# The second product of a ReLU-squared layer by tile pairs: half of its depth plainly, half as seven quarter products

## The chip, the cores and the metric

One core of a Trainium2 chip. The metric is the device time of one execution in microseconds (us). In the text TensorE is PE (its weight loads PEld), VectorE is DVE, ScalarE is ACT, GpSimd is POOL, and SP is the engine whose queue starts most transfers.

## What is computed

Windowed attention with sinks, then a layer with a gated softmax and a normalization, then a last layer. The change touches the last layer:

```python
def _moe2_ref(x, w_in, w_out):        # x 1536 x 512, w_in 512 x 2048, w_out 2048 x 512
    h = x @ w_in
    r = np.maximum(h, 0.0)
    g = r * r
    return (g @ w_out).astype(np.float32)   # the second product
```

Everything is fp32, to be kept nearly exactly. A product of two fp32 matrices is made of three matmuls in the format fp32r: each operand is split into a rounded part (hi) and the rest (lo), and hi x hi, hi x lo and lo x hi are summed in PSUM.

## The kernel before

The kernel runs on hand-written queues: each engine has its own list of instructions, in the order of the program text of its block, and semaphores tie them together. There is no scheduler; whatever stands behind a waiting instruction of the same engine waits too.

The attention and the middle layer take the first 200 us. Then comes the first product of the last layer, transposed: `g` has the shape [128, NJ = 8, 2, 1536], where chunk (j, r) is the 128 rows 128 x (8r + j) of `g` transposed. The first two j are made of plain quarters (`quarter`), the six others (`multiply`, j = 2 to 7) as seven products each with 384 columns: the scheme multiplies a 2 x 2 block matrix with seven products instead of eight, at the price of sums of blocks. Each of these seven products is 12 matmuls. DVE adds its results (`sum_2`, `sum_3`, `lower_right`, `lower_left`, `upper_right`), ACT copies two of them (`copy_p1`, `corner`), and DVE applies max and square (`gate_row`, L1559). POOL sums and splits the weights of that product (L791 to L805) and has nothing to do after it.

The second product, `project2` (L2014 to L2034), takes 12 tiles of 128 tokens. For a tile t, the 16 chunks of `g` are the stationary operand, and `wy`, the split w_out, the moving one, with 512 columns: 16 x 3 = 48 matmuls add up one PSUM bank. ACT rounds a whole tile of g (`round_g`, L1141) into one of two buffers `g_hi`, DVE subtracts to get `g_lo` (`split_g`, L1573), two tiles ahead. The eight pairs of chunks of w_out are loaded, rounded by ACT (`round_wy`, L1132) and split by DVE (`split_wy`, L1563) around the change from the first product to the second. The first two tiles are done in turns of four chunks, so that TensorE can begin before all of `wy` is there. Finished banks are copied by ACT (even tiles) or DVE (odd ones) into `y`, and SP stores them. The last tile's bank is copied by DVE in two halves (L1581, L1582), the second of which ACT's own queue stores (L1212).

TensorE's operand order is plain there:

```python
for k in range(3):
    gs, w = ((g_hi, 0), (g_hi, 1), (g_lo, 0))[k]
    done = mm(y_ps[t % 8], gs[t % 2][:, n, :], wy[n // 2][:, n % 2, w, :], ...)
```

## Time and profile before

| | us |
|---|---|
| median of 3 runs | 476.38 (475.81 to 476.69) |
| the profiled execution | 474.66 |
| its span, first to last instruction | 472.9 |
| TensorE busy | 462.9 |
| VectorE busy | 303.9 |
| ScalarE busy | 213.7 |
| GpSimd busy | 126.0 |
| granted TensorE clock, mean | 0.999 |

The profile is one execution, so times inside it are compared with its own 474.66. A matmul's recorded duration contains its way through the array; successive matmuls overlap, and what a matmul costs in a stream is the distance between starts. Loads of weights (PEld) overlap matmuls. The same holds, to a smaller degree, for the other engines: an instruction starts some 0.08 us before the record of the one before it ends. In a line of the timeline "x2" means that two like instructions are shown as one, from the first start to the last end. Idle time of an engine that is not on the chain costs nothing.

### The profile page before, as it was taken

Reading aid. Unit: us, or ns where it says so; the run is one execution under the profiler, and the core shown is the slowest. Engines: PE = TensorE matmul, PEld = TensorE weight load, DVE = VectorE, ACT = ScalarE, POOL = GpSimd, SP = SyncE. Lnnn points to the kernel's source line nnn. Section 1 sums busy time; section 2 is a strip of 40 time slices with the busy share of each in tenths; the row PEclk is TensorE's granted clock in tenths of the full one; section 3 lists DMA queues with packets and bytes.
Section 4 is the critical chain, followed back from the end, with each engine's and each line's share of the span. In section 5 each row is a group of like instructions: output and inputs, shape, how many; then the busy total and the mean of one; then the engine's idle time right before and its main releaser. Section 6 shows DMA issues by size and latency. Waiting matters only on the chain.

```text
span 472.9 us, 7375 instructions
## 1 busy us (share of the span) xinstructions
PE 462.9 (98%) x2754; PEld 395.4 (84%) x2754; DVE 303.9 (64%) x491; ACT 213.7 (45%) x538; POOL 126.0 (27%) x175
## 2 busy tenths in 40 slices
PE   8889999999999999999999999999999999999997
PEld 6667787887778887788999999999988888888885
DVE  3899888998898889874863766557974121212120
ACT  4687777656866576444554122222533212122210
POOL 2366333231311330512444576551000000000000
PEclk9999999999999999999999999999999999999999
DMA  7921124543564855464301111011511000000010
GB/s 225 326 85 48 52 71 138 169 126 78 162 169 130 189 134 156 110 152 117 91 1 46 44 46 46 0 44 49 191 73 45 23 22 24 22 24 22 22 46 22
DMA packets 60443, 41.87 MB, mean 89 GB/s; under 512 B 28344, under 2 KB 48056, under 8 KB 60408
## 3 DMA queue, kind: packets, MB, share of 16 engines
q1 hardware_dynamic: 59640, 40.74, 30.7%
q10 hardware_dynamic: 768, 0.66, 0.5%
q8 instruction: 22, 0.36, 0.3%
q14 instruction: 13, 0.11, 0.1%
HBM read 30.38 MB, written 11.01 MB: 88 GB/s over the span
## 4 chain that ended last, share of the span: by engine, by line
PE 90%; DVE 3%; POOL 3%; ACT 2%; issue 1%; DVEq 0%; POOLq 0%
PE wo_ps L1816 13%; PE h_ps L1776 12%; PE wt_ps L2031 9%; PE score_ps L2031 9%; PE score_ps L1978 7%; PE h_ps L2010 5%; PE score_ps L2010 5%; PE wo_ps L2031 5%; PE h_ps L2031 5%; PE wo_ps L2010 4%; PE wt_ps L2010 4%; PE wo_ps L1738 3%; PE score_ps L1704 3%; PE wt_ps L1704 1%; POOL pT_own L697 1%; PE wt_ps L1715 1%
## 5 line engine op out<-in xcount | busy, mean ns | idle before, releaser
L1573 DVE TENSOR_TENSOR g_lo<-g,g_hi 128x2048 fp32r<-128x2048 f32 (+2 forms) x14 | 27.7, 1986 | 76.4 <-ACT g_hi L1141 75.2
L1141 ACT ACTIVATE g_hi<-g 128x2048 fp32r<-128x2048 f32 (+2 forms) x14 | 23.3, 1671 | 84.9 <-PE score_ps L2031 25.2
L2031 PE MATMUL wt_ps<-wy,g_hi 128*128 128x512 f32 x128 | 39.7, 391 | 0.0
L2031 PE MATMUL score_ps<-wy,g_hi 128*128 128x512 f32 x128 | 39.7, 391 | 0.0
L882 ACT ACTIVATE prob<-sm,nbias 128x132 f32<-128x132 f32 (+1 forms) x96 | 37.7, 394 | 3.7 <-DVE nbias L1231 3.0
L1816 PE MATMUL wo_ps<-wo_hi,lnT_hi 128*128 128x512 f32 x88 | 36.1, 411 | 0.0
L1776 PE MATMUL h_ps<-w_hi,xT_hi 128*128 128x512 f32 x88 | 35.3, 401 | 0.8 <-DVE xT_lo L1340 0.5
L1816 PE MATMUL wo_ps<-wo_hi,lnT_lo 128*128 128x512 f32 x88 | 35.0, 398 | 0.0
L1776 PE MATMUL h_ps<-w_hi,xT_lo 128*128 128x512 f32 x88 | 34.5, 392 | 0.0
L1816 PE MATMUL wo_ps<-wo_lo,lnT_hi 128*128 128x512 f32 x88 | 34.4, 391 | 0.0
L1776 PE MATMUL h_ps<-w_lo,xT_hi 128*128 128x512 f32 x88 | 34.3, 390 | 0.0
L805 POOL TENSOR_TENSOR w_lo<-w_raw,w_hi 128x512 fp32r<-128x512 f32 x16 | 22.1, 1386 | 41.7 <-ACT w_hi L1110 41.7
L2031 PEld LDWEIGHTS wt_ps<-wy,g_hi 128*128 128x128 f32 x128 | 24.0, 188 | 5.2
L2031 PEld LDWEIGHTS score_ps<-wy,g_hi 128*128 128x128 f32 x128 | 24.0, 188 | 5.1
L2031 PE MATMUL wt_ps<-wy,g_lo 128*128 128x512 f32 x64 | 25.1, 392 | 0.0
L2031 PE MATMUL score_ps<-wy,g_lo 128*128 128x512 f32 x64 | 25.0, 390 | 0.0
L687 POOL CAST p_sink<-prob 128x64 fp32r<-128x64 f32 x10 | 4.8, 484 | 75.2 <-DVE prob L1307 75.2
L1559 DVE SCALAR_TENSOR_TENSOR g<-g 128x1536 f32<-128x1536 f32 x12 | 22.9, 1914 | 0.3
L1776 PEld LDWEIGHTS h_ps<-w_hi,xT_hi 128*128 128x128 f32 x88 | 16.5, 188 | 6.8 <-issue 3.5
L1978 PE MATMUL score_ps<-xc_hi,w_hi 128*128 128x384 f32 x64 | 21.5, 337 | 0.0
L1978 PE MATMUL score_ps<-xc_lo,w_hi 128*128 128x384 f32 x64 | 21.5, 336 | 0.0
L1978 PE MATMUL score_ps<-xc_hi,w_lo 128*128 128x384 f32 x64 | 21.5, 336 | 0.0
(231 smaller groups left out, 1263.0 us busy)
## 6 DMA issues: line engine op xcount, KB each, us to landing
u_dram<-uT SPq DMA_DIRECT2D x18, 256.0 KB, 3.3
lnT_raw<-u_dram SPq DMA_DIRECT2D x36, 128.0 KB, 2.8
w_raw<-w_in SPq DMA_DIRECT2D x16, 256.0 KB, 3.3
V<-v SPq DMA_DIRECT2D x12, 256.0 KB, 3.3
wy_in<-w_out SPq DMA_DIRECT2D x6, 512.0 KB, 4.0
x_dram<-x SPq DMA_DIRECT2D x44, 64.0 KB, 2.2
out<-y SPq DMA_DIRECT2D x11, 256.0 KB, 2.0
k_raw<-kT SPq DMA_DIRECT2D x20, 132.0 KB, 2.8
```

What stands on the lines that cost most here:

```text
L805: nc.gpsimd.tensor_tensor(w2_slots(w2_lo[j % 2], part), w2_part(j, part), w2_slots(w2_hi[j % 2], part).bitcast(F32), ALU.subtract).then_in ...
L882: nc.scalar.activation(prob[:, h, seen(n)], sm[:, h, seen(n)], ACT.Exp, bias=nbias[:, h:h + 1], scale=-1.0 if alone(n) else SCALE, accum_o ...
L1141: nc.scalar.activation(g_hi[t % 2][:, chunks, :], g_tile(t, chunks), ACT.Copy).then_inc(g_rounded, 1)
L1559: nc.vector.scalar_tensor_tensor(h, h, 0.0, h, ALU.max, ALU.mult).then_inc(g_ready, 1)
L1573: nc.vector.tensor_tensor(g_lo[t % 2][:, chunks, :], g_tile(t, chunks), g_hi[t % 2][:, chunks, :].bitcast(F32), ALU.subtract).then_inc(g_s ...
L1704: done = mm(score_banks(n, p)[:, j, cols], qs[rows], ks[rows], start=(n < 2 or i == 0), stop=(n < 2 or i == len(products) - 1))
L1738: last = mm(o_ps[rows, cols], V[:, slot, h * D:(h + 1) * D], pT[:, g, j * P:(j + 1) * P], start=(g == 0 and part == 0 and i < 2 and not si ...
L1776: done = mm(h_ps[:, cols], xs[:, c, :], ws[:, c, cols], start=(c == 0 and k == 0), stop=(c == MC - 1 and k == 2))
L1816: done = mm(x2_bank(t)[:, :], ls[:, k, :], ws[:, k, :], start=(k == 0 and i == 0), stop=(k == C1 - 1 and i == 2))
L1978: done = mm(quarter_ps[n % 2], ws[j % 2][:, 2 * r + half, cc, :], x(s, xs[half])[:, cc, :], start=(c == 0 and k == 0), stop=(c == MC - 1 a ...
L2010: last = mm(prod_pairs[j % 2][bank][:, s, 0:TH], ws[j % 2][:, wk, c, :], xs[s][xk][:, c, :], start=(opens and c == 0 and k == 0), stop=(c ...
L2031: done = mm(y_ps[t % 8], gs[t % 2][:, n, :], wy[n // 2][:, n % 2, w, :], start=(n == 0 and k == 0), stop=(n == C2 - 1 and k == 2))
```

## The change

The 12 tiles become 6 pairs (p, p + 6). The depth of the product, the eight j, is cut in two.

- The *plain* part of a pair uses j = 0 to 3: four items of 12 matmuls with 512 columns (two tiles x two halves of the chunks), into the pair's two banks `pair_ps[p % 3]`.
- The *seven* part uses j = 4 to 7. Its matrix is cut into quarters: the two tiles of the pair by the two r, and w_out by r and by halves of 256 columns. Seven items of 12 matmuls with 256 columns (4 chunks x 3). In order: FIFTH, FIRST, THIRD, SIXTH, SECOND, SEVENTH, FOURTH. FIFTH has a bank of its own; FIRST, SIXTH and SEVENTH share one (`chain_ps`), which ACT or DVE must have read before the next may open it; the rest adds onto the plain part's banks.
- The order of the parts (`PLAN`) is plain 0, 1, 2, seven 0, plain 3, seven 1, plain 4, seven 2, seven 3, plain 5, seven 4, seven 5: 24 + 42 = 66 items.
- An item's high part is rounded by ACT into a ring of seven buffers of 512 elements, its low part is written by DVE over g itself; both are made seven items ahead.
- POOL makes the four sums of blocks of g of each pair, S1 to S4, of 512 elements each, after the pair's plain part, over the chunks that the plain part has used. DVE waits for two of them before it splits the pair's FIFTH item, and for all four before FIRST.
- Of w_out, j = 0 to 3 are loaded, rounded and split as before. The rest is loaded as four quarters, DVE makes four differences T1 to T4, ACT rounds seven matrices of 1024 elements and DVE splits them, written between the items 0 to 7.
- Of a seven part ACT copies three results (`keep`), DVE adds the others (`flush`) into `y`; SP stores a tile of the pair when DVE has added the last.

```diff
+PLAN = (("plain", 0), ("plain", 1), ("plain", 2), ("seven", 0), ("plain", 3), ("seven", 1),
+        ("plain", 4), ("seven", 2), ("seven", 3), ("plain", 5), ("seven", 4), ("seven", 5))
+PAIR_PRODUCTS = ((S1, T1), (A11, B11), (S4, B22), (S2, T2), (A12, B21), (S3, T3), (A22, T4))
...
+            def sum_g(p, k):
+
+                done = len(WST_SUMS) * p
+                if k == S1:
+                    pool.wait_ge(item_done, item("plain", p, PARTS - 1) + 1)
+                    pool.wait_ge(g_ready, gates_before(NJ))
+                elif k == S2:
+                    pool.wait_ge(s_summed, done + 1)
+                elif k == S4:
+                    pool.wait_ge(s_summed, done + 2)
...
+                nc.gpsimd.tensor_tensor(g_sum(g, p, k), a, b, op).then_inc(s_summed, 1)
...
                 copy_p1(j)
                 if j == NJ - 1:
-                    round_g(0, 0)
+                    for n in range(6):
+                        round_item(n)
                 corner(j)
...
+            for n in range(len(ITEMS)):
+                keep(n)
+                if n + RING < len(ITEMS):
+                    round_item(n + RING)
+                if n == 0:
+                    round_wst(B11)
...
+            def prepare(n):
+
+                kind, p, i = ITEMS[n]
+                if kind == "seven" and i == FIFTH:
+                    dve.wait_ge(s_summed, len(WST_SUMS) * p + 2)
+                elif kind == "seven" and i == FIRST:
+                    dve.wait_ge(s_summed, len(WST_SUMS) * (p + 1))
+                split_item(n)
...
+                if i == SIXTH:
+                    dve.wait_ge(kept, kept_before(p) + 1)
+                    nc.vector.tensor_tensor(upper[:, HALF:DM], chain_ps, lower[:, HALF:DM], ALU.add).then_inc(chain_summed, 1)
...
+            for n in range(len(ITEMS)):
+                flush(n)
+                if n + RING < len(ITEMS):
+                    prepare(n + RING)
+                if n == 1:
+                    sum_wst(T1)
+                    sum_wst(T2)
+                elif n == 2:
+                    split_wst(T1)
+                    sum_wst(T3)
+                elif n == 3:
+                    sum_wst(T4)
+                    split_wst(B11)
+                elif n == 4:
+                    split_wst(B22)
+                    split_wst(T2)
+                elif n == 5:
+                    split_wst(B21)
+                elif n == 6:
+                    split_wst(T3)
+                elif n == 7:
+                    split_wst(T4)
...
+                elif i == SIXTH:
+                    pe.wait_ge(kept, kept_before(p) + 2)
+                elif i == SEVENTH:
+                    pe.wait_ge(chain_summed, 2 * p + 1)
...
+                for c in range(NJ - PLAIN):
+                    for k in range(3):
+                        gs, w = ((item_high(n), 0), (item_high(n), 1), (item_raw(g_low, n), 0))[k]
+                        done = mm(bank, gs[:, c, :], wst[wk][:, w, c, :], start=((i in (FIFTH, FIRST) or bank is last_ps) and c == 0 and k == 0),
+                                  stop=(c == NJ - PLAIN - 1 and k == 2), skip_group_check=True)
```

## Rows read from the trace of the kernel before

**Rows 1.** The page's first part: busy us, share of the span, instructions.

```profile
PE 462.9 (98%) x2754; PEld 395.4 (84%) x2754; DVE 303.9 (64%) x491; ACT 213.7 (45%) x538; POOL 126.0 (27%) x175
```

**Rows 2.** The chain that ended last: start us, us, what (TensorE's two products).

```profile
250.29 2.09 PE score_ps L2010 x12
...
338.01 21.88 PE score_ps L2031 x96
```

**Rows 3.** Busy time by engine from 349 us to the last matmul.

```profile
349.00:469.90 120.90, 120.88 (x528) 98.76 (x527) 28.63 (x18) 23.17 (x18) 0.00 (x0) 1.00 0.07 24
```

**Rows 4.** Timeline, TensorE, matmuls of 260 columns: start us, us, engine, line.

```profile
109.89 0.39 PE L1704 MATMUL score_ps<-KH,QH 64*128 64x260 f32 x2
110.12 0.28 PE L1704 MATMUL score_ps<-KL,QH 64*128 64x260 f32 x2
...
110.47 0.28 PE L1704 MATMUL wt_ps<-KL,QH 64*128 64x260 f32 x2
```

**Rows 5.** Weight loads: two groups by shape (busy us, mean ns | idle), one timeline line.

```profile
L2031 PEld LDWEIGHTS wt_ps<-wy,g_hi 128*128 128x128 f32 x128 | 24.0, 188 | 5.2
...
L1759 PEld LDWEIGHTS wo_ps<-p_sinkT,v_sink 96*128 96x128 f32 x40 | 5.7, 190 | 1.6 <-issue 0.7 <-ACT p_sinkT L900 0.4
...
125.32 0.52 PEld L1759 LDWEIGHTS wo_ps<-p_sinkT,v_sink 96*128 96x128 f32 x4 [0.39 <-issue]
```

**Rows 6.** Timeline, VectorE, an instruction of 512 elements and the next one.

```profile
9.35 0.69 DVE L1307 TENSOR_TENSOR prob<-prob,rz 128x512 f32<-128x512 f32 x1
9.96 0.69 DVE L1472 TENSOR_SCALAR w_hi<-w_stage 128x1024 fp32r<-128x1024 f32 x1
```

**Rows 7.** Groups by shape: line, engine, shapes, count | busy us, mean ns | idle before.

```profile
L1563 DVE TENSOR_TENSOR wy<-wy_ahead,wy 128x1024 fp32r<-128x1024 f32 x2 | 2.4, 1218 | 0.0
...
L1110 ACT ACTIVATE w_hi<-w_sum 128x512 fp32r<-128x512 f32 x6 | 3.7, 622 | 0.0
...
L1126 ACT COPY g<-h_ps 128x768 f32<-128x768 f32 x3 | 2.4, 804 | 7.1 <-PE h_ps L2010 7.1
```

**Rows 8.** Timeline of VectorE and ScalarE at the change of products.

```profile
337.97 2.02 DVE L1573 TENSOR_TENSOR g_lo<-g,g_hi 128x1792 fp32r<-128x1792 f32 x1
338.10 2.01 ACT L1132 ACTIVATE wy<-wy_ahead 128x1024 fp32r<-128x1024 f32 x2 [1.73 <-PE h_ps L2010]
...
339.91 2.35 DVE L1563 TENSOR_TENSOR wy<-wy_ahead,wy 128x1024 fp32r<-128x1024 f32 x2
...
342.18 0.95 DVE L1545 TENSOR_TENSOR g<-h_ps,g 128x768 f32<-128x768 f32 x1
343.05 3.42 DVE L1559 SCALAR_TENSOR_TENSOR g<-g 128x1536 f32<-128x1536 f32 x2
```

**Rows 9.** One line's instructions, L805: ns min/median/max, first and last start us.

```profile
L805 POOL TENSOR_TENSOR w_lo<-w_raw,w_hi x16: 1284/1298/2029, 196.1 to 319.0; 128x512 fp32r<-128x512 f32 x16
```

**Rows 10.** Timeline, GpSimd and VectorE together, both operands of each in SBUF.

```profile
196.13 1.29 POOL L805 TENSOR_TENSOR w_lo<-w_raw,w_hi 128x512 fp32r<-128x512 f32 x1 [2.19 <-ACT w_hi L1110]
...
196.71 1.53 DVE L1522 TENSOR_TENSOR xc_lo<-x2T,xc_hi 128x768 fp32r<-128x768 f32 x1
...
197.38 2.01 POOL L805 TENSOR_TENSOR w_lo<-w_raw,w_hi 128x512 fp32r<-128x512 f32 x1
...
196.71 3.50 DVE L1522 TENSOR_TENSOR xc_lo<-x2T,xc_hi 128x768 fp32r<-128x768 f32 x2
```

**Rows 11.** Timeline, VectorE reading PSUM beside GpSimd.

```profile
265.76 0.94 DVE L1545 TENSOR_TENSOR g<-score_ps,g 128x768 f32<-128x768 f32 x1
266.40 0.74 POOL L799 TENSOR_TENSOR w_last<-w_raw,w_sum 128x256 f32<-128x256 f32 x1
```

**Rows 12.** Timeline of the end: the last copies and ScalarE's store.

```profile
469.92 0.42 DVE L1581 COPY y<-wt_ps 128x256 f32<-128x256 f32 x1 [17.10 <-PE wt_ps L2031]
470.26 0.41 DVE L1582 COPY y<-wt_ps 128x256 f32<-128x256 f32 x1
...
470.71 0.36 ACTq L1212 DMA_DIRECT2D out<-y  x1
```

More of the change, by code:

```diff
@@ L68 @@
 P_FIRST, P_SECOND, P_CORNER, P_THIRD, P_LOWER, P_LEFT, P_RIGHT = range(NP)
-EARLY_TILES = 2
 AHEAD = (2, 3)
-WY_LOADS = AHEAD + (0, 1, 4, 5, 6, 7)
+PLAIN = 4
+WY_LOADS = AHEAD + (0, 1)
+HALF = DM // 2
+NPAIR = NT // 2
+RING = 7
+PLAN = (("plain", 0), ("plain", 1), ("plain", 2), ("seven", 0), ("plain", 3), ("seven", 1),
+        ("plain", 4), ("seven", 2), ("seven", 3), ("plain", 5), ("seven", 4), ("seven", 5))
+PAIR_PRODUCTS = ((S1, T1), (A11, B11), (S4, B22), (S2, T2), (A12, B21), (S3, T3), (A22, T4))
+FIFTH, FIRST, THIRD, SIXTH, SECOND, SEVENTH, FOURTH = range(NP)
+PARTS = PLAIN
+WST_ROUNDS = (B11, B22, T1, T2, B21, T3, T4)
+WST_SPLITS = (T1, B11, B22, T2, B21, T3, T4)
+WST_SUMS = (T1, T2, T3, T4)
 LN_EPS, SM_EPS = 1e-6, 1e-9
@@ L198, in gates_before, with parts_of, kept_before, item @@
     return len(BLOCKS) + 2 * (j - CLASSIC)
+def parts_of(kind):
+    return PARTS if kind == "plain" else NP
+ITEMS = tuple((kind, p, i) for kind, p in PLAN for i in range(parts_of(kind)))
+def kept_before(p):
+    return 3 * p
+def item(kind, p, i):
+    return ITEMS.index((kind, p, i))
 def seen(n):
@@ L841, in _ @@
                 split_w2(j)
+            for p in range(NPAIR):
+                for k in (S1, S2, S3, S4):
+                    sum_g(p, k)
         @block.scalar
@@ new lines, in round_wst, with keep @@
+            def round_wst(k):
+                if k in WST_SUMS:
+                    act.wait_ge(wst_summed, WST_SUMS.index(k) + 1)
+                else:
+                    act.wait_ge(wst_loaded, 16 * 4)
+                nc.scalar.activation(wst[k][:, 0, :, :], wst_raw(k), ACT.Copy).then_inc(wst_rounded, 1)
+            def keep(n):
+                kind, p, i = ITEMS[n]
+                upper, lower = y[2 * (p % 2)], y[2 * (p % 2) + 1]
+                if kind == "plain" or i not in (FIFTH, FIRST, SEVENTH):
+                    return
+                act.wait_ge(item_done, n + 1)
+                if i == FIFTH:
+                    if p >= 2:
+                        act.wait_ge(y_stored[p % 2], 32 * (p // 2))
+                    nc.scalar.copy(lower[:, HALF:DM], fifth_ps).then_inc(kept, 1)
+                elif i == FIRST:
+                    nc.scalar.copy(upper[:, 0:HALF], chain_ps).then_inc(kept, 1)
+                else:
+                    nc.scalar.copy(lower[:, 0:HALF], chain_ps).then_inc(kept, 1)
@@ L1636, in _ @@
                 if last:
[L1637 removed]
+                    split_item(0)
+                    split_item(1)
                 elif j - CLASSIC + 1 < len(BLOCKS):
@@ L1640, in _ @@
                 sum_3(j)
+                if last:
+                    split_item(2)
                 lower_right(j)
@@ new lines, in plain_part @@
+            def plain_part(p, i):
+                n = item("plain", p, i)
+                half, part = i % 2, i // 2
+                pe.wait_ge(item_split, n + 1)
+                if p == 0 and i == 0:
+                    pe.wait_ge(added, 5 * (NJ - 1 - CLASSIC))
+                elif p == 2 and i == 0:
+                    pe.wait_ge(added, 5 * (NJ - CLASSIC))
+                elif p >= 3 and part == 0:
+                    pe.wait_ge(y_summed, 2 * (p - 3) + half + 1)
+                for c in range(4):
+                    j, r = 2 * part + c // 2, c % 2
+                    if p == 0:
+                        pe.wait_ge(wy_split, j + 1)
+                    for k in range(3):
+                        gs, w = ((item_high(n), 0), (item_high(n), 1), (item_raw(g_low, n), 0))[k]
+                        done = mm(pair_ps[p % 3][half], gs[:, c // 2, r, :], wy[j][:, r, w, :],
+                                  start=(part == 0 and c == 0 and k == 0), stop=(part == 1 and c == 3 and k == 2),
+                                  skip_group_check=True)
+                done.then_inc(item_done, 1)
@@ L2047, in _ @@
                     multiply(j, n)
-            for first, last in ((0, 4), (4, 8), (8, C2)):
-                for t in range(EARLY_TILES):
-                    project2(t, first, last)
-            for t in range(EARLY_TILES, NT):
-                project2(t, 0, C2)
+            for kind, p in PLAN:
+                for i in range(parts_of(kind)):
+                    if kind == "plain":
+                        plain_part(p, i)
+                    else:
+                        seven_part(p, i)
 def kernel(q, k, v, n_sink, window, moe_w_in, moe_w_out, moe_g_ln, moe2_w_in, moe2_w_out):
```

245 lines of the change are left out of this document (151 added, 94 removed).

## The prediction

> **What bounds the kernel now.** I read the page's first part, then the chain that ended last, then the second product's stretch, then the engines beside it. TensorE is busy 98% of 472.9 us, GpSimd 27% [rows 1]. The chain is TensorE alone from 250.29 on, and from 338.01 on it is L2031, the second product, in six pieces of 22 us each [rows 2] up to the last copies at 469.92 [rows 12]. From 349 on TensorE is busy 120.88 of 120.90 us at a granted clock of 1.00 (that is 2.4 GHz), while VectorE works 28.6 us, ScalarE 23.2, GpSimd 0 [rows 3]. So a shorter matmul stream shortens the kernel one for one, as long as the three other engines feed it. Their idle time looks ample as an average; it has to be read block by block.
>
> **TensorE's stream.** Before: 576 matmuls of 512 columns in 131.9 us, 0.229 each. After: six pairs with 48 plain matmuls each (288 of 512 columns), and 84 of 256 columns each (504), where plain work would have been 96 of 256. The trace has no 128-row matmul of 256 columns. In the first product, 504 matmuls of 384 columns go from 250.29 to 338.01: 0.174 each, waits every twelve included [rows 2]. A line through 512 and 384 gives 0.119 at 256. The nearest row agrees: 260 columns in 64 rows, two side by side, go on every 0.117 us (110.12 to 110.47 in three steps) [rows 4]. I take 0.119, bounds 0.117 and 0.174 (384 columns). New stream 288 x 0.229 + 504 x 0.119 = 66.0 + 60.0 = 125.9, so **-6.0 us**. Break-even is 65.9/504 = 0.131.
>
> **Weight loads.** Each narrow matmul comes with its own load of 128x128 weights, as wide a load as a 512-column matmul has. A load is recorded at 0.19, of 128 rows as of 96; but loads overlap: four of 96 rows end within 0.52, so (0.52 - 0.19)/3 = 0.11 apart [rows 5]. 0.119 is just above that; what a narrower margin would do is rival 3.
>
> **What DVE has to do before the first seven-product block.** Prices: splitting 512 elements 0.69 alone, the next instruction starts 0.61 later (9.35 to 9.96) [rows 6]; 1024 elements 1.22, two in 2.35, so 1.13 apart [rows 7, 8]; an addition from PSUM of 768 elements 0.95 [rows 7], so about 0.42 for 256 and 0.36 to the next start. The handover: before, split of g 337.97 to 339.99, two wy splits, addition, two gates to 346.47 [rows 8]. After, the long split is one of 0.61; the wy splits wait for ScalarE's first rounding (half of 2.01, so 339.1) and end at 341.4; addition 342.3; three item splits 344.1; gates 347.4. TensorE doesn't notice: the first items were split during the last block of the first product. ScalarE's six roundings put in ahead of the corner copy cost 6 x 0.62 minus overlap, and end near 330.0; the copy (0.80 [rows 7]) ends 330.9, before the fifth product's start at 331.8 (three products of 2.09 before 338.01). Cover 0.9; it costs that much more if gone. On SP's queue four loads of halves of w_out (512 KB each) take the place of the last four of eight, and twelve stores stay twelve; ScalarE asks for the halves after its first item, DVE after 348.6, some ten us after the last of them may start at 338.0. Cover several us; no cost.
>
> From 347.4 DVE runs in its written order. Before TensorE may open the sixth product of pair 0 (SEVENTH, which waits for DVE's addition of SIXTH out of the shared bank) DVE has: 15 item splits (7 to 21) x 0.61 = 9.1; 4 weight sums and 7 weight splits x 1.13 = 12.4; the addition 0.36. Sum 21.9, so 369.3. TensorE wants it at 338.0 + 144 x 0.229 + 60 x 0.119 = 378.1. **Slack 8.8 us** if GpSimd costs DVE nothing.
>
> **GpSimd's sums.** 24 additions of 512 elements, four per pair: nearest row L805, 512 elements of the same stride pattern, 1.29 median, 2.03 worst [rows 9]. The worst one is the point. At 196.13 GpSimd starts (1.29, ends 197.42); DVE starts a two-input split of 768 at 196.71 and takes 1.53 where 0.95 is usual, ending 198.24: 0.82 after GpSimd. GpSimd's next starts at 197.38, takes 2.01, ends 199.39: 1.15 after DVE. DVE's second ends at 200.21 (196.71 + 3.50), again 0.82 after [rows 10]. They take turns, whole instruction by whole instruction. An addition that reads PSUM doesn't take part: 0.94 beside a GpSimd instruction of its usual 0.74 [rows 11]. So one turn of GpSimd costs a full DVE queue 1.15 + 0.82 - 0.87 = **1.10 us** (0.87: start to start of 768 elements, 342.18 to 343.05 [rows 8]). The Trainium skill (GPSIMD Engine Reference, section Key points) says the two share SBUF interfaces and contend when the Vector instruction has two SBUF inputs; the trace agrees and gives the price, which the page doesn't.
>
> *Block seven 0.* Pairs 0, 1, 2 have their sums released when plain 0, 1, 2 end (349, 360, 371): all 12 fall in DVE's full stretch. 12 x 1.10 = 13.2 against 8.8 of slack: **+4.4 us**. At 1.0 a turn +3.2, at 1.30 +6.8, below 0.73 nothing.
>
> *Blocks seven 1 and seven 2* follow a plain part whose sums are released at the same moment. With 0 there: sum 1.4, split 2.0, sum 3.1, split 3.7, sum 4.8, split 5.4, sum 6.5, split 7.05, addition of SIXTH 7.45; TensorE wants it at 5 x 1.43 = 7.15. **+0.3 each** (0 to 1.2). *Seven 3* has no sums beside it. *Seven 4*: DVE's split for pair 5's FIRST waits for all four sums of pair 5 (queued behind that wait on DVE: the later splits and seven 4's own addition of SIXTH, on which TensorE waits). Sums end 6.0, two splits 7.3, addition 7.7: **+0.6** (0.3 to 1.5).
>
> After a stop the first matmul comes on 0.23 instead of 0.12 later (109.89, 110.12 [rows 4]): 0.11 x 4 = **+0.4**. DVE's additions otherwise replace copies of similar length, with 22 us of slack per pair.
>
> *Tail.* Before: two DVE copies in a row (469.92, 470.26 for 0.41), then ScalarE issues the store at 470.71 [rows 12], 0.8 after the last matmul. After: one addition, ready when the last product ends or up to 0.3 later (ScalarE copy, then 0.42 and 0.69 behind SEVENTH, against 1.43). **-0.1** (-0.3 to +0.3).
>
> **Sum.** -6.0 + 4.4 + 0.3 + 0.3 + 0.6 + 0.4 - 0.1 = -0.1 us on the profiled execution: 474.66 (span 472.9, 1.7 around it) to 474.6. That execution is 1.7 below the median of the three runs, 476.38, within the few tenths of a per cent by which runs differ; on the median the forecast is **476.3 us**: no change that can be measured (0.2% is 0.95 us, about what a measurement of this kernel can tell).
>
> **Rivals.**
> 1. *The turns cost little* (GpSimd's sums slip in where DVE waits anyway, or a waiting GpSimd instruction is passed over until DVE stops). For it: GpSimd isn't needed early for pairs 1 and 2. Against: rows 10. With 0.9 a turn, seven 0 stops 2.0 and the later ones vanish: -6.0 + 2.0 + 0.2 - 0.1, 472.5; with none, -6.1: 470.3.
> 2. *The turns cost more: slower.* Place: seven 0. If a turn costs the whole 1.30, stops are 6.8 + 1.2 + 1.2 + 1.5, restarts 0.4: +5.0, 481.4; half way +2.5, 478.8. It decides from a turn of 1.19 on (12 x 0.09 more than forecast). For it: dependent sums wait for each other's semaphores. Against: between two sums DVE has a turn, which covers that.
> 3. *Narrow matmuls are bound by their loads: slower.* If a load of 128 rows went on in proportion to rows, 0.11 x 128/96 = 0.147: 504 x 0.147 = 74.1, +8.2 against before, partly under the stops: +9, 485. Against: a load of 96 rows and one of 128 are recorded alike, 190 and 188 ns [rows 5]. The Trainium skill (TensorE: Matmul & The Clock Gate, section LDWEIGHTS) says that a load's time goes by its columns alone, 107 ns for 128, which no row here shows for 128 rows; by it this rival falls away.
> 4. *The change doesn't do what it says*: that the rewritten stream isn't run as written (say both halves still plain) is excluded by the diff; that the weights' halves come late to pair 0 is inside the forecast, since their eleven instructions stand in the same DVE queue and their stop is the one counted. No chance of its own.
>
> **How the numbers follow.** Forecast case 0.50 (474.8 to 478.0 on the median; of it 0.14 faster, 0.25 same, 0.11 slower); rival 1 0.27, all faster; rival 2 0.18, slower; rival 3 0.05, slower. Faster 0.41, same 0.25, slower 0.34. The range reaches into rival 1 down to 471.2 and into rival 2 up to 479.8, leaving about 0.1 at either end.
>
> **What would show it.** Steps right: 512-column matmuls every 0.229 and 256-column ones every 0.119; DVE nearly unbroken from 347 to 382, its splits stretched from 0.69 to 1.8 wherever GpSimd runs; TensorE idle about 4 us within the first seven-product block, waiting on DVE, a few tenths in the second, third and fifth, none in the fourth. Wrong: GpSimd's sums waiting long and bunched (rival 1), TensorE's narrow matmuls at 0.13 or more without waits (rival 3), a granted clock that drops during the stops.

## The result, and the profile after

The changed kernel takes 478.0 us in the median (476.62 to 480.29, 12 runs), the kernel before 475.94 (474.81 to 477.26, 12 runs). The ratio is 1.0045, with a 95% interval of 1.0028 to 1.0063: slower by 2.1 us, where no change was forecast. The profiled execution of after took 479.0 us (span 477.2), that of before 474.66 (span 472.9).

Of the 4.3 us between those two spans, 2.1 lie ahead of the second product, whose first matmul starts at 337.84 us in the trace of before and at 339.96 in that of after. That is no effect of the change: in the fifteen traces of this study that moment lies anywhere from 337.75 to 339.96, and the lowest is that of e7 below, which differs from after only inside the second product. So from here on I compare L, the time from the first matmul start of the second product to the last. It is 131.65 us before and 134.0 after. With the tail (last matmul start to the end of the span, 3.43 and 3.27) that makes +2.2 us, against +2.1 by the medians.

The page's line of engine times, which answers [rows 1]:

```profile
PE 460.7 (97%) x2970; PEld 403.2 (84%) x2970; DVE 356.5 (75%) x568; ACT 235.6 (49%) x605; POOL 167.6 (35%) x199
```

TensorE has 2.2 us less work, and is the bound for a smaller share. Busy time by engine, as in [rows 3], from 349 us to the last matmul, and then within the first seven-product block (columns: PE, PEld, DVE, ACT, POOL, each with its count; granted clock; DMA share; GB/s):

```profile
349.00:474.20 125.20, 119.78 (x754) 107.61 (x752) 83.82 (x95) 45.44 (x80) 41.78 (x24) 1.00 0.06 24
372.90:387.90 15.00, 11.03 (x85) 10.23 (x84) 14.37 (x17) 5.24 (x10) 7.72 (x4) 1.00 0.05 17
```

TensorE idles 5.4 us in the first of these, 4.0 of them in the block, where VectorE is busy 14.4 of 15.0. (A matmul's record reaches into the gap behind it, so idle time by records is a little under the stops by starts that I give below.) The granted clock is 1.00 (2.4 GHz) all along. The waits from 335 us to the end put the idle time on VectorE (engine, line, waited for: us, times, longest):

```profile
PEld wo_ps L2245 <- DVE g_low L1692: 6.3, 5, 2.4
...
PE wo_ps L2245 <- DVE y L1733: 3.2, 4, 1.7
```

The chain that ended last, which answers [rows 2], is no longer TensorE alone. It runs through VectorE's weight sums and splits and then its item splits (start us, us, what):

```profile
358.14 2.32 DVE wst_in L1715
366.18 4.56 DVE wst L1720 x2
...
379.74 4.78 DVE g_low L1692 x6
388.12 11.20 PE score_ps L2214 x48
...
409.95 11.20 PE wt_ps L2214 x48
```

TensorE at the entry of block seven 0 and at its two large stops (timeline):

```profile
372.92 0.40 PE L2245 MATMUL wo_ps<-wst,ring 128*128 128x256 f32 x2
373.15 0.28 PE L2245 MATMUL wo_ps<-wst,g_low 128*128 128x256 f32 x1
...
379.87 0.50 PE L2245 MATMUL wo_ps<-wst,ring 128*128 128x256 f32 x2 [2.20 <-DVE g_low L1692]
...
385.01 0.47 PE L2245 MATMUL wo_ps<-wst,ring 128*128 128x256 f32 x2 [1.74 <-DVE y L1733]
```

By the starts of all narrow matmuls between two stops they come every 0.120 us (the first two take 0.23 here, 372.92 to 373.15): [rows 4] was a good neighbour. The stops are in the block that the forecast named. Split over the block by the starts of the matmuls they are 0.19, 2.36, 0.16 and 1.90: 4.6 us. They stand ahead of THIRD, SIXTH, SECOND and SEVENTH. The forecast had all of it ahead of SEVENTH; more than half comes two items earlier, where SIXTH waits for its own low part, which stands in the same late VectorE queue.

VectorE and GpSimd in the stretch before (timeline), which answers [rows 6] and [rows 10]:

```profile
351.19 8.19 POOL L896 TENSOR_TENSOR g<-g 128x512 f32<-128x512 f32 x4 [28.09 <-PE score_ps L2214]
...
354.19 1.78 DVE L1692 TENSOR_TENSOR g_low<-g,ring 128x512 fp32r<-128x512 f32 x1
355.90 2.31 DVE L1720 TENSOR_TENSOR wst<-wst_in,wst 128x1024 fp32r<-128x1024 f32 x1
358.14 2.32 DVE L1715 TENSOR_TENSOR wst_in<-wst_in,wst_in 128x1024 f32<-128x1024 f32 x1
360.38 0.68 DVE L1692 TENSOR_TENSOR g_low<-g,ring 128x512 fp32r<-128x512 f32 x1
```

Beside GpSimd, a split of 512 takes 1.71 from start to start (354.19 to 355.90) where alone it takes 0.61, and one of 1024 takes 2.24 (355.90 to 358.14) where alone it takes 1.13. The differences are 1.10 and 1.11: a turn costs the same whatever VectorE's instruction is, and costs what the forecast said. The block's sum holds too. VectorE ended the gates at 349.68, and its addition of SIXTH at 384.86:

```profile
346.26 3.42 DVE L1681 SCALAR_TENSOR_TENSOR g<-g 128x1536 f32<-128x1536 f32 x2
...
384.45 0.41 DVE L1733 TENSOR_TENSOR y<-wo_ps,y 128x256 f32<-128x256 f32 x1
```

That is 35.2 us; the forecast had 21.9 of work and 13.2 of turns, 35.1.

What the forecast didn't have is in the plain parts. Two rows of plain 1, ahead of any narrow block, and two of plain 3, which follows block seven 0; in each pair the second starts six matmuls after the first:

```profile
360.33 0.39 PE L2214 MATMUL wt_ps<-wy,g_low 128*128 128x512 f32 x1
...
361.70 0.39 PE L2214 MATMUL wt_ps<-wy,g_low 128*128 128x512 f32 x1
...
396.12 0.40 PE L2214 MATMUL score_ps<-wy,g_low 128*128 128x512 f32 x1
...
397.52 0.40 PE L2214 MATMUL score_ps<-wy,g_low 128*128 128x512 f32 x1
```

Six matmuls of 512 columns take 1.37 us ahead of the first narrow block and 1.40 behind it. Over all 144 on either side that is 0.229 each (32.96 us by the starts) against 0.2333. The chain says the same with all 48 of a part: 11.20 us, where 96 of before took 22.00 and so 48 took 11.0. All three plain parts that follow a narrow block run so, 144 matmuls; the three ahead of it run at 0.229.

Blocks seven 1, seven 2 and seven 4 stop once each, at the same place, ahead of SEVENTH. VectorE's addition of SIXTH in seven 1, the same in seven 4, and TensorE behind the latter:

```profile
406.29 0.41 DVE L1733 TENSOR_TENSOR y<-wo_ps,y 128x256 f32<-128x256 f32 x1
...
460.49 0.42 DVE L1733 TENSOR_TENSOR y<-wo_ps,y 128x256 f32<-128x256 f32 x1
...
461.05 0.47 PE L2245 MATMUL wo_ps<-wst,ring 128*128 128x256 f32 x2 [0.79 <-DVE y L1733]
```

By the starts of the matmuls the stops are 0.49 (seven 1), 0.49 (seven 2) and 0.95 (seven 4), and none in seven 3 and seven 5. The tail, which answers [rows 12]:

```profile
474.57 0.42 DVE L1746 TENSOR_TENSOR y<-score_ps,y 128x256 f32<-128x256 f32 x1
475.03 0.36 ACTq L1334 DMA_DIRECT2D out<-y  x1
```

### The profile page after: what moved, and what is told of

Its sections match the earlier page's. It is cut to its first block, busy times and chain, and to the rows that moved or that the text cites. A ratio compares the mean times of both kernels' runs of the same rounds, so it can differ in the third digit from the quotient of the medians.

```text
span 477.2 us, 8100 instructions
## 1 busy us (share of the span) xinstructions
PE 460.7 (97%) x2970; PEld 403.2 (84%) x2970; DVE 356.5 (75%) x568; ACT 235.6 (49%) x605; POOL 167.6 (35%) x199
## 4 chain that ended last, share of the span: by engine, by line
PE 68%; DVE 14%; DMA 5%; POOL 4%; issue 4%; SPq 3%; ACT 2%; POOLq 0%; DVEq 0%; ACTq 0%
PE h_ps L1959 10%; PE wo_ps L1999 10%; PE score_ps L2161 7%; PE h_ps L2193 5%; PE score_ps L2193 5%; PE wo_ps L2245 5%; PE wo_ps L2193 4%; PE wt_ps L2193 4%; DVE g_low L1692 4%; PE h_ps L2214 2%; PE wt_ps L2214 2%; PE score_ps L2214 2%; PE wo_ps L1921 2%; DVE wst L1720 2%; DMA V<-v 2%
## 5 line engine op out<-in xcount | busy, mean ns | idle before, releaser
L1692 DVE TENSOR_TENSOR g_low<-g,ring 128x512 fp32r<-128x512 f32 x66 | 57.2, 881 | 31.8 <-ACT ring L1239 29.0
L896 POOL TENSOR_TENSOR g<-g 128x512 f32<-128x512 f32 x24 | 41.8, 1762 | 94.2 <-PE score_ps L2214 46.5
L1239 ACT ACTIVATE ring<-g 128x512 fp32r<-128x512 f32 x66 | 40.5, 629 | 49.3 <-PE h_ps L2214 14.6
L2245 PE MATMUL wo_ps<-wst,ring 128*128 128x256 f32 x192 | 35.7, 285 | 5.4 <-DVE y L1733 3.2
L1959 PE MATMUL h_ps<-w_hi,xT_hi 128*128 128x512 f32 x88 | 35.2, 400 | 1.5 <-DVE xT_lo L1462 1.2
L2245 PEld LDWEIGHTS wo_ps<-wst,ring 128*128 128x128 f32 x192 | 30.1, 191 | 6.6 <-DVE g_low L1692 6.3
L2245 PE MATMUL wo_ps<-wst,g_low 128*128 128x256 f32 x96 | 27.1, 283 | 0.0
L1000 ACT ACTIVATE e<-h_ps,nhmax 128x512 f32<-128x512 f32 x24 | 16.3, 685 | 10.8 <-DVE nhmax L1383 10.7
L2214 PE MATMUL wt_ps<-wy,ring 128*128 128x512 f32 x64 | 20.1, 395 | 0.0
```

The costliest lines, as they stand in the source:

```text
L896: nc.gpsimd.tensor_tensor(g_sum(g, p, k), a, b, op).then_inc(s_summed, 1)
L1239: nc.scalar.activation(item_high(n), item_raw(g, n), ACT.Copy).then_inc(item_rounded, 1)
L1692: nc.vector.tensor_tensor(item_raw(g_low, n), item_raw(g, n), item_high(n).bitcast(F32), ALU.subtract).then_inc(item_split, 1)
L1959: done = mm(h_ps[:, cols], xs[:, c, :], ws[:, c, cols], start=(c == 0 and k == 0), stop=(c == MC - 1 and k == 2))
L2214: done = mm(pair_ps[p % 3][half], gs[:, c // 2, r, :], wy[j][:, r, w, :], start=(part == 0 and c == 0 and k == 0), stop=(part == 1 and c = ...
L2245: done = mm(bank, gs[:, c, :], wst[wk][:, w, c, :], start=((i in (FIFTH, FIRST) or bank is last_ps) and c == 0 and k == 0), stop=(c == NJ ...
```

## The experiments

My theory after the result: GpSimd's sums take 1.10 us each from VectorE's queue; this stops TensorE 6.5 us, and 0.6 us more go to restarts behind the stops (the first matmuls of a product that comes after a stop stand 0.07 to 0.1 further apart). Without the stops the new order of work gains what its matmuls give. Rivals: the seven-product blocks are slow for a reason of their own (weights late, banks, order), or GpSimd's sums are themselves the late operand. Each kernel is the kernel after with the edit shown, unless it says otherwise. Ratios are against the kernel before, run beside it. This is what came out:

| kernel | median us | ratio (95%) | L, us | stops, us |
|---|---|---|---|---|
| after | 478.0 | 1.0045 (1.0028 to 1.0063) | 134.0 | 4.6, 0.49, 0.49, 0.95 |
| e1 sums of 1 element | 470.96 | 0.9893 (0.9874 to 0.9912) | 126.91 | none |
| e2 sums of 256 | 470.92 | 0.9892 (0.9869 to 0.9914) | 126.91 | none |
| e7 sums of 384 | 471.88 | 0.9927 (0.9902 to 0.9952) | 128.64 | 1.67 |
| e8 copies of 512 | 470.98 | 0.9909 (0.9893 to 0.9925) | 126.91 | none |
| e5 sums on VectorE | 471.19 | 0.9905 (0.9879 to 0.9931) | 126.91 | none |
| e3 sums released later | 472.64 | 0.993 (0.9911 to 0.9948) | 128.54 | 0.55, 0.94 |
| e4 later, other plan | 471.31 | 0.992 (0.9888 to 0.9951) | 127.53 | 0.54 |
| e9 short weight splits | 472.99 | 0.9945 (0.9932 to 0.9959) | 129.61 | 0.49, 0.49, 0.49, 0.95 |
| e6 each sum twice | 498.98 | 1.0491 (1.0463 to 1.052) | 154.83 | 20.2 in all |

**e1: GpSimd's sums cut to one element.** The splits of the items that would read a sum read g itself.

```diff
-                nc.gpsimd.tensor_tensor(g_sum(g, p, k), a, b, op).then_inc(s_summed, 1)
+                nc.gpsimd.tensor_tensor(g_sum(g, p, k)[:, 0:1, 0:1], a[:, 0:1, 0:1], b[:, 0:1, 0:1], op).then_inc(s_summed, 1)
```

> Leaves out the pairs' sums of g: each of GpSimd's 24 instructions works on one element per partition instead of 512, and the items that used the sums take a quarter of g in their place (same sizes, same waits). Theory 1 (turns: GpSimd's two-input instructions and VectorE's with both inputs in SBUF take turns, 1.1 us each, which makes VectorE's queue late): all stops of TensorE in the four blocks (4.6, 0.5, 0.5, 0.95 us) and their restarts (0.5) vanish, the 512-element splits are back at 0.69 us: 478.0 - 7.0 = 471.0, ratio to the kernel before 0.990. Rival A (VectorE's own queue, 11 weight instructions and 15 splits, is too long, GpSimd or not): the stops in the first block stay, 477 or more. Rival B (ScalarE's roundings come late): as rival A.

470.96 us, and every stop is gone: L is 126.91. All of the 7.1 us between this and after (134.0 - 126.91) hang on the length of GpSimd's sums; with short sums, weights, banks and the order of the plan stop TensorE nowhere. The plain parts behind narrow blocks stay at 0.2333, so that has nothing to do with the length of GpSimd's sums.

**e2 and e7: 256 and 384 of the 512 elements.** Does the price go by the size of GpSimd's instruction? As in e1, the items that would read a sum read g. The edit of e2 (e7 has 96 in place of P // 2):

```diff
-                nc.gpsimd.tensor_tensor(g_sum(g, p, k), a, b, op).then_inc(s_summed, 1)
+                nc.gpsimd.tensor_tensor(g_sum(g, p, k)[:, :, 0:P // 2], a[:, :, 0:P // 2], b[:, :, 0:P // 2], op).then_inc(s_summed, 1)
```

> As the run with one element, but each of GpSimd's sums covers 256 of the 512 elements (so half of each sum is left out). Theory 1: a turn of 256 elements costs VectorE 0.55 us, 12 x 0.55 = 6.6 us are less than the 8.8 us of slack before the first seven-product block's SEVENTH, so no stop there, and at most 0.1 to 0.3 in the last: 471.0 to 471.4, the same as with one element. A rival in which the loss goes in proportion to GpSimd's work (bandwidth of the memory shared by all instructions, say) gives half of the loss: 474.5.

> As the runs with shortened sums, but 384 of the 512 elements (a quarter of each sum left out). Theory 1: a turn costs VectorE (0.55 + 1.10)/2 = 0.82 us, 12 x 0.82 = 9.9 us against 8.8 of slack: one stop of 1.1 to 1.5 us in the first seven-product block, nothing else over 0.3: 471.0 + 1.5 = 472.4. It is the point just past the bend; a loss in proportion to GpSimd's elements would give 471.0 + 3/4 x 7.0 = 476.2.

256 elements: no stop, 470.92. VectorE's timeline in e2 has two instructions that start 1.68 us apart instead of 1.13, so a turn costs 0.55:

```profile
353.76 1.76 DVE L1722 TENSOR_TENSOR wst<-wst_in,wst 128x1024 fp32r<-128x1024 f32 x1
355.44 1.75 DVE L1717 TENSOR_TENSOR wst_in<-wst_in,wst_in 128x1024 f32<-128x1024 f32 x1
```

384 elements: one stop of 1.67 us ahead of SEVENTH in block seven 0, 471.88 us, a little under what was expected. VectorE's timeline in e7:

```profile
353.12 2.04 DVE L1722 TENSOR_TENSOR wst<-wst_in,wst 128x1024 fp32r<-128x1024 f32 x1
355.09 2.03 DVE L1717 TENSOR_TENSOR wst_in<-wst_in,wst_in 128x1024 f32<-128x1024 f32 x1
```

From start to start 1.97 instead of 1.13: a turn costs 0.84 here, against 1.10 for 512. Twelve are 10.1, 1.3 more than the slack of 8.8. The stop is 1.67 with the 0.3 us by which the handover came later than forecast. So the time bends where the slack puts the bend: between 256 and 384 elements.

**e8: a copy in place of each sum.** One input instead of two, 512 elements; the sums are left out, as in e1.

```diff
-                nc.gpsimd.tensor_tensor(g_sum(g, p, k), a, b, op).then_inc(s_summed, 1)
+                nc.gpsimd.tensor_copy(g_sum(g, p, k), a).then_inc(s_summed, 1)
```

> The kernel after with each of GpSimd's 24 sums replaced by a copy of its first operand, 512 elements, one input in place of two (the sums of g are left out; the split of these items reads g itself). Counts, places and waits stay. If a one-input instruction of GpSimd takes turns with VectorE too, at about half the price (0.55 a turn, as the sum of 256 elements had), 12 turns cost 6.6 us of the 8.8 in hand: no stop, 471.0 to 471.4 us, but VectorE's splits beside the copies are still longer than their 0.69 alone. If it takes no turn: the same time, and the splits take 0.69 us throughout. If it costs a full turn as the two-input one does: the stops stay, 478 us.

470.98 us. GpSimd and VectorE in its timeline:

```profile
350.22 5.45 POOL L898 COPY g<-g 128x512 f32<-128x512 f32 x4 [28.07 <-PE score_ps L2216]
...
352.73 0.91 DVE L1694 TENSOR_TENSOR g_low<-g,ring 128x512 fp32r<-128x512 f32 x1
353.56 1.63 DVE L1722 TENSOR_TENSOR wst<-wst_in,wst 128x1024 fp32r<-128x1024 f32 x1
355.11 1.63 DVE L1717 TENSOR_TENSOR wst_in<-wst_in,wst_in 128x1024 f32<-128x1024 f32 x1
```

A one-input instruction disturbs VectorE too, but less: 353.56 to 355.11 is 1.55 instead of 1.13, so 0.42, and 352.73 to 353.56 is 0.83 instead of 0.61, so 0.22, where 0.55 was expected. "No stop" came from the smaller price. The 0.22 stands alone; the four turns of the next pair's copies (361.87 to 367.01) cost 0.41 or 0.42 each. The price becomes plain beside the time that GpSimd's instruction takes when nothing is in its way. Its least, median and largest time in ns, in after, e7, e2 and e8:

```profile
L896 POOL TENSOR_TENSOR g<-g x24: 1297/1736/2283, 351.2 to 457.4; 128x512 f32<-128x512 f32 x24
L898 POOL TENSOR_TENSOR g<-g x24: 1003/1463/2005, 349.0 to 450.0; 128x384 f32<-128x384 f32 x24
L898 POOL TENSOR_TENSOR g<-g x24: 731/1132/1722, 350.2 to 448.6; 128x256 f32<-128x256 f32 x24
L898 POOL COPY g<-g x24: 609/842/1610, 350.2 to 448.4; 128x512 f32<-128x512 f32 x24
```

The least times are 1.30, 1.00, 0.73 and 0.61 us, the prices 1.10, 0.84, 0.55 and 0.42: each is the instruction's own least time less 0.16 to 0.20. So the copy takes a whole turn as the sums do, and is cheaper because it is shorter. (In e1 the least time is 0.18, and no price is left.)

**e9: VectorE's weight splits shortened, GpSimd untouched.** This tells "VectorE's queue is too long" from "GpSimd's sums are late".

```diff
-                nc.vector.tensor_tensor(wst[k][:, 1, :, :], wst_raw(k), wst[k][:, 0, :, :].bitcast(F32), ALU.subtract
+                nc.vector.tensor_tensor(wst[k][:, 1, 0:1, 0:1], wst_raw(k)[:, 0:1, 0:1], wst[k][:, 0, 0:1, 0:1].bitcast(F32), ALU.subtract
...
-                        gs, w = ((item_high(n), 0), (item_high(n), 1), (item_raw(g_low, n), 0))[k]
+                        gs, w = ((item_high(n), 0), (item_high(n), 0), (item_raw(g_low, n), 0))[k]
```

> The kernel after, in which the seven subtractions on VectorE that form the low part of the weights of the quarter products are cut to one element, and the second of each three matmuls reads the high part of the weights again (the low part of these weights is left out of the product; the count and the shapes of the matmuls stay). GpSimd's sums are untouched. It takes about 7 x 1.1 = 7.8 us out of VectorE's queue ahead of block seven 0, with no change to GpSimd. Theory (a GpSimd sum of 512 elements costs VectorE one turn of 1.10 us, and the sums stop TensorE only where 12 turns, 13.2 us, exceed VectorE's slack, then 8.8 + 7.8 = 16.6 us): the stops of block seven 0 (4.6 us) and its restarts (0.2 to 0.3) go, those of seven 1, 2 and 4 (0.49, 0.49, 0.95) stay: 478.0 - 4.8 = 473.2 us (472.7 to 473.7). Rival: GpSimd's sums themselves come too late for block seven 0, whatever VectorE carries: the stops there stay, 478 us. Second rival: VectorE's load has nothing to do with turns, and the same stops shrink by less than half: 475.5 to 477.

472.99 us. The stops of block seven 0 shrink from 4.6 to one of 0.49, the others stay to the hundredth. So the first block's stop is the length of VectorE's queue. The expectation had nothing left in seven 0; what is left is the later blocks' mechanism, since pair 2's sums are released as the block begins, and it is as large as there.

**e3 and e4: the same sums, released later.** e3 delays the release of pairs 2, 3 and 4; e4 delays pair 5's too, and puts plain 5 ahead of seven 3, so that no block stands beside sums that it needs soon.

```diff
+RELEASE = {2: 18, 3: 29, 4: 38}
...
-                    pool.wait_ge(item_done, item("plain", p, PARTS - 1) + 1)
+                    pool.wait_ge(item_done, max(item("plain", p, PARTS - 1), RELEASE.get(p, 0)) + 1)
```

> Computes everything. Only the moment changes from which GpSimd may make a pair's sums: pair 2 after item 18 (end of the first seven-product block) instead of 11, pair 3 after 29 instead of 22, pair 4 after 38 instead of 33. Theory 1: 8 turns instead of 12 fall in VectorE's full stretch, 8 x 1.1 = 8.8 us, just the slack: the first block's 4.6 us go to 0 to 0.5, those of the second and third (0.5 each) vanish, the last keeps 0.95: 478.0 - 4.6 - 1.0 - 0.4 = 472.0 (to 472.6), ratio 0.992. Rivals A and B: same GpSimd work, same VectorE and ScalarE work, so no change: 478.

```diff
+RELEASE = {2: 18, 3: 29, 4: 40, 5: 48}
...
-        ("plain", 4), ("seven", 2), ("seven", 3), ("plain", 5), ("seven", 4), ("seven", 5))
+        ("plain", 4), ("seven", 2), ("plain", 5), ("seven", 3), ("seven", 4), ("seven", 5))
```

> Computes everything. As the run with later sums, and plain 5 stands before seven 3 instead of behind it, with pair 4's sums from item 41 on and pair 5's from item 49 on, so that no block of seven products begins beside its own release of sums. Theory 1: the last stop (0.95) goes as well; pair 0 to 1 as before (0.55): 472.6 - 1.0 = 471.6.

472.64 and 471.31 us. In e3, two stops are left: 0.55 in seven 0 (eight turns are 8.8, all of the slack, and the handover was late) and 0.94 in seven 4, untouched by this edit. In e4 only the first is left (0.54).

The work is all there; only its moment moved, and 5.4 and 6.7 us came back. GpSimd's sums were not wanted as early as they were released.

**e5: the sums on VectorE.** Each of the 24 sums is put into VectorE's order, ahead of the item before which it is needed; GpSimd does none.

```diff
+DVE_SUMS = {4: ((0, S1), (0, S2)), 5: ((0, S3), (0, S4)), 8: ((1, S1), (1, S2)), 9: ((1, S3), (1, S4)),
+            18: ((2, S1), (2, S2)), 19: ((2, S3), (2, S4)), 30: tuple((3, k) for k in (S1, S2, S3, S4)),
+            40: tuple((4, k) for k in (S1, S2, S3, S4)), 52: tuple((5, k) for k in (S1, S2, S3, S4))}
...
-                nc.gpsimd.tensor_tensor(g_sum(g, p, k), a, b, op).then_inc(s_summed, 1)
+                nc.vector.tensor_tensor(g_sum(g, p, k), a, b, op).then_inc(s_summed, 1)
...
+                for p, k in DVE_SUMS.get(n, ()):
+                    sum_g(p, k)
                 flush(n)
```

> Computes everything. The 24 sums move from GpSimd to VectorE's queue, four per pair, at items 4 and 5, 8 and 9, 18 and 19, 30, 40, 52. Theory 1: a sum on VectorE costs it 0.61 us where the same sum on GpSimd costs it a turn of 1.10; the eight before the first block's SEVENTH cost 4.9 of 8.8 us of slack: no stop but at most 0.3 in the block of the last pair but one: 471.2, ratio 0.990. Rival A (VectorE's queue is too long by itself): it gets 24 instructions more, so slower than the changed kernel, 480 or more.

471.19 us, 0.9905 of before (0.9879 to 0.9931) and 6.8 us under after: a version that beats both. Its groups for the item splits and for the sums, by shape, from 335 us on (busy us, mean ns | idle before):

```profile
L1676 DVE TENSOR_TENSOR g_low<-g,ring 128x512 fp32r<-128x512 f32 x63 | 42.5, 688 | 28.1 <-ACT ring L1223 27.6
...
L1693 DVE TENSOR_TENSOR g<-g 128x512 f32<-128x512 f32 x24 | 15.7, 686 | 0.2
```

The same two groups in after:

```profile
L1692 DVE TENSOR_TENSOR g_low<-g,ring 128x512 fp32r<-128x512 f32 x64 | 55.9, 887 | 31.8 <-ACT ring L1239 29.0 <-POOL g L896 2.4
...
L896 POOL TENSOR_TENSOR g<-g 128x512 f32<-128x512 f32 x24 | 41.8, 1762 | 94.2 <-PE score_ps L2214 46.5 <-PE h_ps L2214 29.0 <-PE wt_ps L2214 18.2
```

A sum costs VectorE 0.61 from start to start when it does it itself, and 1.10 when GpSimd does it beside a full VectorE queue. Handing it over cost more than it took away.

**e6: each sum twice.** The opposite dose: 48 sums of 512 elements.

```diff
+                nc.gpsimd.tensor_tensor(g_sum(g, p, k), a, b, op).then_inc(s_again, 1)
+                pool.wait_ge(s_again, done + (S1, S2, S3, S4).index(k) + 1)
                 nc.gpsimd.tensor_tensor(g_sum(g, p, k), a, b, op).then_inc(s_summed, 1)
```

> Computes everything; each of GpSimd's 24 sums is made twice, one after the other. Theory 1: twelve turns more in VectorE's full stretch, 13.2 us, if all come before the first block's SEVENTH; the second and third block hardly change (four splits there can meet four turns, one kind or the other), the fifth waits for 5.3 us more of sums: about +4.9. 478.0 + 13.2 + 4.9 = 496.1, range 490 to 500. If the stops weren't due to turns but to the moment at which a pair's sums are finished (data, not VectorE's queue): only the fifth block, 483.

498.98 us: 2.9 above the value expected, inside its bounds. The stops alone are a little less than that. VectorE's addition of SIXTH in seven 0 ends 46.9 us after the gates (348.91 to 395.86), 11.7 later than in after; twelve more turns would make 13.2, but the last of the 24 sums comes too late to delay it. The stop of seven 4 is 6.07, about as expected (0.95 + 4.9). Above the expected value lies what follows these two blocks' last stops, of 6.1 us each: matmuls of 256 columns come every 0.213 us instead of 0.12, some 13 of them in seven 0 and some 25 in seven 4, which costs 1.4 and 2.6 us. The same pace stands earlier in seven 0, between its stops, where it costs nothing more, since TensorE waits there for VectorE anyway. Busy time and granted clock in three stretches of block seven 0 of e6, and in one behind the stop of seven 4 (columns as above; the clock is the third number from the end):

```profile
374.00:378.00 4.00, 1.80 (x14) 1.60 (x14) 4.00 (x3) 0.90 (x2) 3.92 (x3) 1.00 0.00 0
378.00:382.00 4.00, 2.41 (x14) 2.12 (x14) 4.00 (x3) 0.90 (x2) 3.92 (x3) 0.56 0.00 0
382.00:386.00 4.00, 3.03 (x14) 2.73 (x14) 4.00 (x3) 0.63 (x1) 3.92 (x3) 0.50 0.00 0
...
478.00:482.00 4.00, 3.40 (x16) 3.43 (x17) 2.25 (x5) 0.89 (x3) 0.00 (x0) 0.50 0.17 66
```

In block seven 0 the clock is granted at 0.50, 1.2 GHz, after the second stop, and in seven 4 at the end of a single one, of 6.07 us. In after, with 4.0 us of idle time in 15, it stayed at 1.00, so this price is no part of its miss.

**c1 to c4: the pace of 0.2333.** These four are the kernel before with extra matmuls of 256 columns put in, whose result is overwritten. The term they test is 144 x 0.0043 = 0.62 us of the miss. c1 puts 12 ahead of tile 5.

```diff
+                    if t == 5 and n == 0:
+                        for extra in range(12):
+                            mm(o_ps[:, 0:DM // 2], g_hi[t % 2][:, extra, :], wy[extra // 2][:, extra % 2, 0, 0:DM // 2],
+                               start=True, stop=True)
                     for k in range(3):
```

> The kernel before with twelve extra matmuls of 256 columns (results not used) ahead of its sixth tile. It asks whether the plain matmuls' 0.2333 us after a block of narrow ones, against 0.2290 ahead of it, comes from the narrow ones. If it does and stays: tiles 5 to 11, 336 matmuls, at 0.2333: 336 x 0.0043 = 1.4 us, plus twelve at 0.12: 475.9 + 1.4 + 1.4 = 478.8. If it comes from the changed kernel's other work (splits over g, the ring): 0.2290 throughout, 477.4.

477.4 us (1.0024, 1.0002 to 1.0045). By the time alone this is the case in which narrow matmuls change nothing; the trace says otherwise. The pace of 0.2333 does appear in a kernel that otherwise never shows it, and ends again: by the starts, 24 matmuls of tile 5 at 0.2333, then ten or so unsteady ones and a steady 0.227. The chain of c1 has tile 5 alone, 11.08 where 11.00 is usual:

```profile
382.57 11.00 PE h_ps L2035 x48
394.99 11.08 PE h_ps L2035 x48
```

c2 makes the burst four times as long (48).

> The kernel before with 48 added matmuls of 256 columns ahead of the twelfth-to-last... tile 5 of the second product (their result is overwritten), four times as many as the burst of 12, after which 25 of the 512-column matmuls were taken at 0.2333 us and the rest at 0.229. If the slower pace lasts in proportion to the narrow matmuls ahead (about 2 for each), some 100 of the 336 that follow run at 0.2333: 476.2 + 48 x 0.118 + 100 x 0.0043 = 482.3 us. If it lasts some 25 matmuls whatever the burst, 482.0 us. If from a longer burst on it lasts to the end, all 336: 483.3 us. The trace tells these apart by the starts of the matmuls; the times hardly can.

481.57 us (1.0122, 1.0106 to 1.0137), and again just 24 matmuls at the slow pace, 11.08 for the tile. The length of the burst doesn't matter:

```profile
394.20 5.70 PE wo_ps L2031 x48
399.90 11.08 PE h_ps L2035 x48
```

Twenty-four matmuls are half a tile, the half that reads the weight tiles wy0 to wy3; the other half reads wy4 to wy7. The kernel after has only wy0 to wy3 in its plain parts. c4 has the burst of 12 and lets tiles 5 to 11 read wy0 to wy3 only; c3 has the burst in the middle of tile 5, ahead of wy4.

```diff
-                        done = mm(y_ps[t % 8], gs[t % 2][:, n, :], wy[n // 2][:, n % 2, w, :],
+                        done = mm(y_ps[t % 8], gs[t % 2][:, n, :], wy[n // 2 % (8 if t < 5 else 4)][:, n % 2, w, :],
```

> The kernel before with the burst of 12 matmuls of 256 columns ahead of tile 5, and tiles 5 to 11 reading the weight tiles wy0 to wy3 twice in place of wy0 to wy7 (the upper half of the weights is left out of these tiles). In the bursts of 12 and of 48 the pace of 0.2333 lasted 24 or 25 matmuls, just those that read wy0 to wy3, and ended where wy4 came; the kernel after reads wy0 to wy3 alone in its plain parts. Theory A (the slow pace is set off by a narrow matmul and lasts until the weight tiles read change to others): all 336 matmuls of tiles 5 to 11 at 0.2333, a stream of 78.4 us, and 475.9 + 1.4 + 336 x (0.2333 - 0.2280) = 479.1 us. Theory B (it lasts some 24 matmuls, or to half the tile, whatever they read): 24 of 336 at 0.2333 and the rest at 0.2266 to 0.2296, 477.4 to 477.9 us.

```diff
-                    if t == 5 and n == 0:
+                    if t == 5 and n == 8:
```

> The kernel before with the same burst of 12 narrow matmuls in the middle of tile 5, ahead of the 24 matmuls that read wy4 to wy7. Theory A1 (narrow matmuls slow whatever follows): the next 24 run at 0.2333 in place of 0.2266, and those of tile 6 as before. Theory A2 (only the stream from wy0 to wy3 has a slower pattern to fall into): the next 24 stay at 0.2266, tile 6's first 24 at 0.2296. Both give 477.3 to 477.6 us; the starts in the trace tell them apart.

c4 takes 478.6 us (1.0061, 1.0034 to 1.0089), c3 477.42 (1.0049, 1.0016 to 1.0083). The chain of c4 to the end, then the piece of c3's behind its burst:

```profile
395.52 11.20 PE h_ps L2035 x48
406.73 22.40 PE wo_ps L2035 x96
...
451.53 22.41 PE wt_ps L2035 x96
```

```profile
400.69 5.45 PE h_ps L2035 x24
406.14 22.00 PE wo_ps L2035 x96
```

In c4 all 336 matmuls that follow 12 narrow ones run at 0.2333 (22.40/96), to the end of the kernel. In c3 the 24 that follow run at 0.227 (5.45/24). So the slow pace is set off by narrow matmuls, only in a stream that reads wy0 to wy3, and lasts until other weight tiles are read: theory A and A2. c1 and c4 differ in nothing but the weight tiles, so it isn't the chunks of g. That reading wy0 to wy3 alone isn't slow by itself is shown by plain 0 to 2 of after, at 0.229. The expected time of c4, 479.1, was 0.5 too high, since I subtracted a pace of 0.2280 where before's chain gives 22.00/96 = 0.2292; with that it is +1.4 +1.4, 478.7. Why these tiles have a second, slower pattern and the others not, the runs don't show.

## Why the prediction was wrong, point by point

Right were the block, the cause and the size of the main stop:
- *The bound and the handover.* TensorE's stream sets the time wherever the others feed it: L is 126.91 us in each of the four kernels without a stop (e1, e2, e5, e8), and apart from e6 each stop adds its own length and 0.07 to 0.10 to that. The handover came 0.3 later than forecast (gates end 9.7 after the product's start, not 9.4).
- *The price of a turn.* 1.10 forecast from [rows 8] and [rows 10], 1.10 and 1.11 measured. Twelve turns and the rest of VectorE's queue were forecast at 35.1 us and took 35.2. Stops in seven 0: 4.4 forecast, 4.6 measured, though not all ahead of SEVENTH, where the forecast put them: 2.36 of it came ahead of SIXTH.
- *Rivals.* Rival 1 (a turn costs little) is refuted by these rows, and by e1 against after: 7.0 us hang on the sums. Rival 2 was placed in seven 0 with turns of 1.19 and more; they are 1.10, so this slower result isn't its mechanism. Rival 3 is refuted: 0.120 for a narrow matmul, in streams without any wait.

Wrong were the sizes of the terms, all in one direction:

| term, us | forecast | measured |
|---|---|---|
| TensorE's stream, without stops | -6.0 | -4.9 |
| stop in seven 0 | +4.4 | +4.6 |
| stops in seven 1, 2, 4 | +0.3, +0.3, +0.6 | +0.49, +0.49, +0.95 |
| restarts | +0.4 | +0.56 |
| tail, beyond the narrower last matmul | -0.1 | about 0 |
| sum | -0.1 | +2.2 |

The measured stream is L of e1, 126.91, against 131.65, and 0.11 for the narrower last matmul, which L leaves out and the tail holds.

- *The step that failed most is TensorE's stream* (1.1 of the 2.3). Its 0.119 for 256 columns came from a line through 384 and 512 columns and was 0.120: 504 x 0.001 = 0.5. And its 0.229 for 512 columns was taken as a constant, a mean over a stream that read eight weight tiles; in the new stream half of these matmuls ran at 0.2333: 0.62. The bounds of 0.117 and 0.174 for the narrow ones were wide enough; for the 512-column ones I gave none, as if the change couldn't touch them. A sum that comes to -0.1 as the difference of two terms near 5 doesn't bear that.
- *The stops of the later blocks* (0.73 of it). In seven 1 VectorE's addition was forecast to end 7.45 after the block's start, and ended 7.54 after it (399.16 to 406.70). TensorE wanted it at 7.2; to that come the handover to TensorE and the load of the next weights, 0.14, which I hadn't counted at any stop. In seven 4 the addition ended 8.0 after the block's start, not 7.7 (452.90 to 460.91).
- *The restarts* were 0.56 us instead of 0.4: seven stops, not four.

None of these is large; together they move the time from "no change" to slower by 0.45%, within the range of 471.2 to 479.8. The forecast case's own range, 474.8 to 478.0, just holds it.

## What to carry to other kernels

Before work goes to GpSimd, price it in VectorE's time: beside a full VectorE queue with operands in SBUF, a two-input sum of 512 elements cost VectorE 1.10 us, more than the 0.61 of doing it itself. The price was GpSimd's own undisturbed time less about 0.2 us, for sums of three sizes and for a copy. So hand work over only where VectorE has slack, and release it no earlier than needed. Where the gain and the cost of a change nearly cancel, give every pace of the main stream its own bounds, also that of the instructions that stay, and let the chance of a miss by two or three small terms of one sign decide between "same" and "slower".
